# Second layer's first product by one level of Strassen's algorithm, with the output product one step behind

## The chip, the cores and the metric

The kernel runs on one core of a Trainium2 chip. A time is the device time in microseconds of one execution. The kernel before took 958.43 us (median of three runs, 956.42 to 958.74). TensorE is called PE, VectorE DVE, ScalarE ACT, GpSimd POOL and SyncE SP, as in the profile; PEld is PE's loading of weights.

## What is computed

A gated linear recurrence over 1536 tokens gives x (1536 x 320). A first layer multiplies it by w_in (320 x 2048), applies a piecewise quadratic function and multiplies by w_out. The second layer, with eight experts that all see all tokens, takes most of the time:

```python
logits = x @ w_gate                      # 1536 x 8
P = np.exp(logits - logits.max())
for _ in range(8):                       # Sinkhorn rounds
    P /= P.sum(1, keepdims=True) + 1e-09
    P /= P.sum(0, keepdims=True) + 1e-09
    P *= N / E
for e in range(E):
    h = np.maximum(x @ w1[e], 0.0)       # first product, 320 x 1024 weights
    out += P[:, e:e + 1] * (h @ w2[e])   # output product, 1024 x 320 weights
```

## The kernel before

Every float32 operand of a large product is held as two parts, hi (rounded to PE's fast 32-bit format) and lo (the rest), and a product is three products: hi x hi, lo x hi, hi x lo. ACT makes the hi parts, DVE or POOL subtract them from the values for the lo parts.

**First layer.** The tokens go in four groups g of 384. For each of 16 slices f of the hidden units PE runs `first_product` (L1221, eight matmuls of 384 columns, L1232) and, two slices behind, `second_product` (L1235, nine of 320 columns, L1242 and L1246). In between DVE clamps (L927), ACT squares (L534), DVE takes the larger (L952), ACT rounds to `ht_hi` (L415) and DVE or POOL make `ht_lo` (L940, L597). Between the slices of groups 0 to 2 stands attention work of the next group. After a group its outputs are copied to `xs`, transposed (`turn_mlp`, L1092) and split into `xt_hi` and `xt_lo`. In the last group PE also computes the router's logits of nine token tiles (`gate_logits`, L1268), and ACT and POOL already split the first expert's weights.

**Second layer.** Work goes by expert and by token group g of 512 (three). One `group` (L1361) on PE is: four times `hidden_pair` (L1334), each 30 matmuls of 512 columns that use 64 rows of the array, in pairs side by side (the 320 inputs are five pieces of 64; copies with swapped halves, `swap_hi` and `swap_lo`, put each piece also into the other half of the rows); then four times `output_tile` (L1348), each 24 matmuls of 320 columns for 128 tokens. ACT applies the relu from PSUM into `h_hi` (L568), DVE makes `h_lo` (L1033) and accumulates each output tile into `acc`, weighted by `prob` (L1050; L1045 for expert 0, whose sums are scaled later by L1041). POOL subtracts for the experts' weights only (`piece_lo_part`, L597). Weights arrive by 64 DMAs of 320 KB on SP's queue (`load_piece`, L316), each when a buffer of `raw` is free; the order on every engine is written out by hand, with semaphores between. The maximum of the logits and the eight Sinkhorn rounds (`sinkhorn_rows` L1000, `sinkhorn_columns` L1015 on DVE, `sum_columns` L1332 on PE) stand between the tiles of expert 0.

```python
for i, (w, x) in enumerate(parts):
    for j in range(2):
        half = slice(j * HALF, (j + 1) * HALF)
        ins = mm(ps_h2[pair % 2 * 2 + j][:, :], w[half, :], x[half, :], ...)
```

Of the kernel before, what the change touches and what calls it, by code (L numbers as in the profile page):

```python
# [22 lines left out]
GT = 3  # L23
# [18 lines left out]
EARLY = 6
SLOTS = 2
RESTS = 8
# [6 lines left out]
def column_round(g, t):  # L51

    r = (g - 1) * T2 + t
    return r if 0 <= r < SINKHORN else None
# [15 lines left out]
def build(nc, gates, select, qk, rows, up_down, rest, pieces, wgate, consts, factors, out):  # L70
# [18 lines left out]
    cst = sb("cst", [P, P + 1 + GH])  # L89
    ident = cst[:, 0:P]  # L90
    mask_up = cst[:, P:P + 1]
    onehot = cst[0:GH, P + 1:P + 1 + GH]
    all_ones = sb("all_ones", [P, P])
    xt_hi = sb("xt_hi", [P, 3, TOK], f32r)
    xt_lo = sb("xt_lo", [P, 3, TOK], f32r)
    before_hidden = mark[0]
# [15 lines left out]
    raw = sb("raw", [P, SLOTS, PU])  # L112
    after_raw = mark[0]
    mark[0] = raw_at
    st_hi = sb("st_hi", [P, RESTS, PS], f32r)
# [3 lines left out]
    wg2 = sb("wg2", [P, 3, 2, E], f32r)  # L119
    xs = sb("xs", [P, GT, 3 * P])  # L120
# [12 lines left out]
    e1_hi = sb("e1_hi", [P, NP2 * PU], f32r)  # L133
    e1_lo = sb("e1_lo", [P, NP2 * PU], f32r)
    h_hi = sb("h_hi", [P, FT2, GN2], f32r)
    h_lo = sb("h_lo", [P, FT2, GN2], f32r)
# [6 lines left out]
    assert mark[0] <= end_mlp  # L143
# [9 lines left out]
    e0_hi = sb("e0_hi", [P, NP2 * PU], f32r)  # L153
    e0_lo = sb("e0_lo", [P, NP2 * PU], f32r)
    swap_hi = sb("swap_hi", [P, 2, TOK], f32r)
    swap_lo = sb("swap_lo", [P, 2, TOK], f32r)
    assert mark[0] <= nc.sbuf_usable_end, (mark[0], nc.sbuf_usable_end)
    ex_hi, ex_lo = (e0_hi, e1_hi), (e0_lo, e1_lo)
# [35 lines left out]
    ps_gate = bank[0]  # L194
    ps_top = bank[1]
    ps_cols = bank[1][:, 2 * P:2 * P + E]
    ps_h2 = (bank[6], bank[7], bank[2], bank[3])
    ps_out2 = bank[4:6]
    ps_turn2 = (bank[6], bank[7], bank[2])
# [16 lines left out]
    piece_in = [mk(f"piece_in{i}") for i in range(SLOTS)]  # L216
    piece_hi = mk("piece_hi")
    piece_split = mk("piece_split")
    swap_in = [mk(f"swap_in{i}") for i in range(2)]
# [32 lines left out]
    wg_ready = mk("wg_ready")  # L252
# [31 lines left out]
    xm_hi = mk("xm_hi")  # L284
# [14 lines left out]
    h2 = mk("h2")  # L299
    hi2 = mk("hi2")  # L300
    lo2 = mk("lo2")
    out2 = mk("out2")
# [5 lines left out]
    waited = mk("waited")  # L308
# [3 lines left out]
    with block:  # L312

        @block.sync
        def _(sp):
            def load_piece(q, i):  # L316

                sp.wait_ge(piece_split, q + 1)
                sp.sem_inc(waited, 1)
                sp.dma_start(raw[:, i, :], pieces[ds(q, 1), :, :].rearrange("a p n -> p (a n)")).then_inc(piece_in[i], 16)  # L320
# [66 lines left out]
            def swap_halves(k, a, b):  # L387

                sp.wait_ge(xm_ready, after(b - 1))
                cols = slice(a * P, b * P)  # L390
                for x, y in ((xt_hi, swap_hi), (xt_lo, swap_lo)):
                    sp.dma_start(y[0:HALF, :, cols].bitcast(f32), x[HALF:P, 0:2, cols].bitcast(f32)).then_inc(swap_in[k], 16)
                    sp.dma_start(y[HALF:P, :, cols].bitcast(f32), x[0:HALF, 0:2, cols].bitcast(f32)).then_inc(swap_in[k], 16)

            sp.wait_ge(m_split, FT1)
            for q in range(NP2 - SLOTS):
                load_piece(q, q % SLOTS)
            swap_halves(0, 0, EARLY_X)
            for q in range(NP2 - SLOTS, NP2 + SLOTS):
                load_piece(q, q % SLOTS)  # L400
            swap_halves(1, EARLY_X, U)
            with sp.Fori((NP2 + SLOTS) // 2, E * NP2 // 2) as i:
                for j in range(2):
                    load_piece(i * 2 + j, j)
            for t in range(U):
                sp.wait_ge(acc_ready, after((E - 1) * U + t))
                row = t % B * S + t // B * P
                sp.dma_start(out[row:row + P, :], acc[:, t, :]).then_inc(stored, 16)
# [4 lines left out]
        def _(act):  # L413
# [3 lines left out]
            def piece_hi_part(q2, i, hi, c):  # L417

                act.wait_ge(piece_in[i], q2 * 16 + 16)
                copy(hi[:, c * PU:(c + 1) * PU], raw[:, i, :]).then_inc(piece_hi, 1)  # L420
# [91 lines left out]
            def copy_mlp(g):  # L512

                for t in range(GT - 1):
                    act.wait_ge(out1, g * GT + t + 1)
                    copy(xs[:, t, 0:DM], ps_out[t][:, 0:DM])
                    copy(xs[:, t, DM:3 * P], ps_out[t][:, 2 * P:DM]).then_inc(x2_act, 1)

            def turn_mlp_hi(g, banks=ps_out):
                for t in range(GT):  # L520
                    turn_hi(xm_turned, g * GT + t, banks[t], g * GN + t * P, xm_hi)

            def mlp(g, first, attention, piece):
                if not first:
                    copy_mlp(g - 1)
                for f in range(FT1 + 2):
# [9 lines left out]
                    if not first and f == 0:  # L536
                        turn_mlp_hi(g - 1)
# [13 lines left out]
            def expert0_piece_at(f):  # L551
                if f % 2 == 0 and f >= 2:
                    q = f // 2 - 1
                    if q == 0:
                        act.wait_ge(xa_ready, after(U - 1))
                    piece_hi_part(q // 2, q % 2, e0_hi, q)
# [4 lines left out]
            mlp(G - 1, False, False, expert0_piece_at)  # L561


            def group(ex, g, nxt, parts, first=False, exp_here=False):

                for f in range(FT2):
                    act.wait_ge(h2, (ex * G2 + g) * FT2 + f + 1)
                    nc.scalar.activation(h_hi[:, f, :], ps_h2[f % 4][:, :], ACT.Relu).then_inc(hi2, 1)  # L568
                    if exp_here and f == 0:
                        act.wait_ge(top_ready, 1)  # L570
                        nc.scalar.activation(prob[:, :, :], prob[:, :, :], ACT.Exp, bias=top[:, 2:3]).then_inc(probs, 1)
                if first:
                    turn_mlp_hi(G - 1, ps_turn2)
                if nxt is not None:
                    for c in parts[g]:
                        piece_hi_part((ex + 1) * (NP2 // 2) + c // 2, c % 2, ex_hi[nxt], c)

            copy_mlp(G - 1)
            for g in range(G2):
                group(0, g, 1, NEXT_FIRST, first=(g == 0), exp_here=(g == 1))  # L580
            for g in range(G2):
                group(1, g, 0, NEXT)
            with act.Fori(1, E // 2 - 1) as ep:
                for slot in range(2):
                    for g in range(G2):
                        group(ep * 2 + slot, g, 1 - slot, NEXT)
            for g in range(G2):
                group(E - 2, g, 1, NEXT)
            for g in range(G2):
                group(E - 1, g, None, NEXT)  # L590

        @block.gpsimd
        def _(pool):
# [3 lines left out]
            def piece_lo_part(q, i, hi, lo, c):  # L599

                pool.wait_ge(piece_hi, q + 1)
                cols = slice(c * PU, (c + 1) * PU)
                sub(lo[:, cols], raw[:, i, :], hi[:, cols].bitcast(f32)).then_inc(piece_split, 1)
# [61 lines left out]
            pool.sem_inc(piece_split, SLOTS)  # L665
# [70 lines left out]
            for ex in range(2):  # L736
                for c in range(NP2):
                    piece_lo_part(ex * NP2 + c, c % 2, ex_hi[ex], ex_lo[ex], c)
            with pool.Fori(1, E // 2) as ep:
                for slot in range(2):  # L740
                    for c in range(NP2):
                        piece_lo_part(ep * (2 * NP2) + slot * NP2 + c, c % 2, ex_hi[slot], ex_lo[slot], c)
# [4 lines left out]
        def _(dve):  # L747
# [5 lines left out]
            for s in (xa_ready, xm_ready, sink, acc_ready):  # L753
                dve.sem_inc(s, FREE)
# [161 lines left out]
            def turn_mlp_lo(g, banks=ps_out):  # L916
                for t in range(GT):
                    turn_lo(xm_hi, g * GT + t, banks[t], g * GN + t * P, xm_ready)

            def mlp(g, first, attention, lo, next_too):  # L920

                for f in range(FT1 + 2):
# [30 lines left out]
                    if f == 0 and not first:  # L953
                        turn_mlp_lo(g - 1)
# [8 lines left out]
                nc.vector.tensor_copy(xs[:, t, 0:DM], ps_out[t][:, 0:DM])  # L963
                nc.vector.tensor_copy(xs[:, t, DM:3 * P], ps_out[t][:, 2 * P:DM]).then_inc(x2_dve, 1)

            mlp(0, True, True, True, True)
# [99 lines left out]
            def no_gate(t):  # L1066
                pass
# [405 lines left out]
```

## Time and profile before

| | us |
|---|---|
| median of three runs | 958.43 |
| profiled execution | 956.86 |
| its span, first to last instruction | 955.1 |
| PE busy | 947.2 |
| DVE busy | 379.5 |
| ACT busy | 254.8 |
| POOL busy | 225.3 |

The profile is of one execution. Busy time is the sum of an engine's instructions; matmuls are pipelined, so the time from the start of one matmul to the start of the next (the spacing) is shorter than its duration. The chain that ended last is followed back from the last instruction, at each step to what released it.

### The profile page before, as it was taken

The page shows a single profiled execution, that of the slowest core. Times are in us where ns is not written, and L with a number is a line of the kernel's source. Part 1 is how long each engine was busy: PE and PEld are TensorE (multiplying, and loading weights), DVE is VectorE, ACT ScalarE, POOL GpSimd, SP SyncE. Part 2 cuts the span into 40 slices and gives each one's busy share as a digit, 9 for nine tenths or more (in the row PEclk, how much of TensorE's full clock was granted, in tenths as well). Part 3 has the DMA queues.
Part 4 walks back from the last instruction along what each step waited for, and adds up shares of the span by engine and source line. Part 5 has one row for each costly group of instructions (what it writes and reads, how often), then busy time and mean ns, then how long its engine had stood idle before and what let it go on. Part 6 is the DMA issues. An engine that isn't in the chain of part 4 may idle for free.

```text
span 955.1 us, 16999 instructions
## 1 busy us (share of the span) xinstructions
PE 947.2 (99%) x7157; PEld 866.3 (91%) x7157; DVE 379.5 (40%) x704; ACT 254.8 (27%) x498; POOL 225.3 (24%) x209
## 2 busy tenths in 40 slices
PE   9999999999999999999999999999999999999998
PEld 7799999999988989889999888999888999988998
DVE  6787665556432654333222222222222222222222
ACT  3544433335432212221212221122222112221111
POOL 5974555441210111110111110111110111110000
PEclk8999999999999999999999999999999999999999
DMA  8723224101611111000110001011001101100000
GB/s 297 228 68 110 76 67 123 43 2 42 154 32 45 42 43 42 27 16 29 42 42 29 28 15 42 29 42 42 29 12 31 42 28 43 41 2 1 29 28 28
DMA packets 29381, 50.38 MB, mean 53 GB/s; under 512 B 2416, under 2 KB 16864, under 8 KB 28928
## 3 DMA queue, kind: packets, MB, share of 16 engines
q1 hardware_dynamic: 28160, 43.59, 15.4%
q10 hardware_dynamic: 1152, 5.77, 1.6%
q8 instruction: 56, 0.92, 0.4%
q14 instruction: 13, 0.11, 0.0%
HBM read 44.15 MB, written 2.05 MB: 48 GB/s over the span
## 4 chain that ended last, share of the span: by engine, by line
PE 93%; DVE 3%; DMA 2%; ACT 1%; SPq 0%; issue 0%; DVEq 0%; ACTq 0%
PE bank L1344 35%; PE bank L1357 35%; PE bank L1232 9%; PE bank L1242 5%; PE bank L1246 3%; PE bank L1157 2%; DMA qk_s<-qk 1%; DMA factors<-dec 1%; PE bank L1130 1%; PE bank L1092 1%; PE bank L1151 1%; DVE ht_lo L940 1%; PE bank L1268 1%; PE bank L1147 0%; DVE h_lo L1033 0%
## 5 line engine op out<-in xcount | busy, mean ns | idle before, releaser
L1357 PE MATMUL bank<-e_hi,h_hi 128*128 128x320 f32 x768 | 241.0, 314 | 0.0
L1357 PE MATMUL bank<-e_lo,h_hi 128*128 128x320 f32 x768 | 237.4, 309 | 0.0
L1357 PE MATMUL bank<-e_hi,h_lo 128*128 128x320 f32 x768 | 237.3, 309 | 0.0
L568 ACT ACTIVATE h_hi<-bank 128x512 fp32r<-128x512 f32 x192 | 104.4, 595 | 469.8 <-PE bank L1344 469.8
L597 POOL TENSOR_TENSOR e_lo<-raw,e_hi 128x640 fp32r<-128x640 f32 x64 | 100.1, 1577 | 545.5 <-ACT e_hi L415 545.5
L1033 DVE SCALAR_TENSOR_TENSOR h_lo<-bank,h_hi 128x512 fp32r<-128x512 f32 x192 | 123.8, 686 | 244.8 <-ACT h_hi L568 244.8
L1357 PEld LDWEIGHTS bank<-e_hi,h_hi 128*128 128x128 f32 x768 | 144.2, 188 | 8.1 <-issue 8.0
L1357 PEld LDWEIGHTS bank<-e_lo,h_hi 128*128 128x128 f32 x768 | 144.3, 188 | 0.0
L1357 PEld LDWEIGHTS bank<-e_hi,h_lo 128*128 128x128 f32 x768 | 144.2, 188 | 0.0
L1050 DVE SCALAR_TENSOR_TENSOR acc<-bank,prob,acc 128x320 f32<-128x320 f32 x84 | 46.3, 551 | 216.5 <-PE bank L1357 216.5
L1344 PE MATMUL bank<-xt_hi,e_hi 64*128 64x512 f32 x576 | 118.0, 401 | 0.1
L1344 PE MATMUL bank<-xt_hi,e_lo 64*128 64x512 f32 x576 | 115.4, 391 | 0.0
L1344 PE MATMUL bank<-xt_lo,e_hi 64*128 64x512 f32 x576 | 114.9, 389 | 0.0
L1344 PE MATMUL bank<-swap_hi,e_lo 64*128 64x512 f32 x384 | 77.1, 392 | 0.0
L1344 PE MATMUL bank<-swap_hi,e_hi 64*128 64x512 f32 x384 | 76.9, 391 | 0.0
L1344 PE MATMUL bank<-swap_lo,e_hi 64*128 64x512 f32 x384 | 76.5, 389 | 0.0
L1344 PEld LDWEIGHTS bank<-xt_hi,e_hi 64*128 64x128 f32 x576 | 55.6, 184 | 15.3 <-issue 4.6
L1344 PEld LDWEIGHTS bank<-xt_hi,e_lo 64*128 64x128 f32 x576 | 55.8, 184 | 11.4
L1344 PEld LDWEIGHTS bank<-xt_lo,e_hi 64*128 64x128 f32 x576 | 55.8, 184 | 10.9
L927 DVE TENSOR_SCALAR vhalf<-bank 128x384 f32<-128x384 f32 x64 | 35.4, 553 | 63.8 <-PE bank L1232 62.3
L415 ACT ACTIVATE e_hi<-raw 128x640 fp32r<-128x640 f32 x64 | 45.0, 740 | 58.8 <-DMA raw<-pieces 58.8
L534 ACT ACTIVATE vhalf<-vhalf 128x384 f32<-128x384 f32 x64 | 33.6, 526 | 85.9 <-DVE vhalf L927 85.9
(134 smaller groups left out, 1139.1 us busy)
## 6 DMA issues: line engine op xcount, KB each, us to landing
raw<-pieces SPq DMA_DIRECT2D x64, 320.0 KB, 2.9
rw<-rows SPq DMA_DIRECT2D x12, 480.0 KB, 6.8
qk_s<-qk SPq DMA_DIRECT2D x12, 416.0 KB
fb<-factors SPq DMA_DIRECT2D x9, 512.0 KB, 5.9
m_raw<-up_down ACTq DMA_DIRECT2D x2, 1440.0 KB, 9.9
result<-acc SPq DMA_DIRECT2D x12, 160.0 KB, 1.8
decb<-factors SPq DMA_DIRECT2D x18, 80.0 KB
m_raw<-up_down ACTq DMA_DIRECT2D x1, 1152.0 KB, 11.2
```

Of the source, the lines that this page charges most:

```text
L415: return nc.scalar.activation(o, i, ACT.Copy)
L534: nc.scalar.activation(vhalf[:, f % 2, :], vhalf[:, f % 2, :], ACT.Square, bias=0.5, scale=0.5).then_inc(sq1, 1)
L568: nc.scalar.activation(h_hi[:, f, :], ps_h2[f % 4][:, :], ACT.Relu).then_inc(hi2, 1)
L597: return nc.gpsimd.tensor_tensor(o, a, b, ALU.subtract)
L927: nc.vector.tensor_scalar(vhalf[:, f % 2, :], ps_h[f % 2][:, 0:GN], -1.0, 1.0, ALU.max, ALU.min).then_inc(clamped, 1)
L1033: stt(h_lo[:, f, :], ps_h2[f % 4][:, :], 0.0, h_hi[:, f, :].bitcast(f32), ALU.max, ALU.subtract).then_inc(lo2, 1)
L1050: stt(acc[:, tile, :], ps_out2[t % 2][:, 0:DM], p, acc[:, tile, :], ALU.mult, ALU.add).then_inc(acc_ready, 1)
L1232: last = mm(dst[:, 0:GN], w, x, start=(i == 0), stop=(i == len(parts) - 1))
L1242: mm(ps_out[t][:, 0:DM], ht_hi[:, slot, t * P:(t + 1) * P], w[:, col:col + DM], start=(first and w is hi), stop=False)
L1246: ins = mm(ps_out[t][:, 0:DM], ht_lo[:, slot, t * P:(t + 1) * P], hi[:, col:col + DM], start=False, stop=last)
L1344: ins = mm(ps_h2[pair % 2 * 2 + j][:, :], w[half, :], x[half, :], start=(i == 0), stop=(i == len(parts) - 1))
L1357: ins = mm(ps_out2[t % 2][:, 0:DM], h[:, f, t * P:(t + 1) * P], w[:, col:col + DM], start=(f == 0 and i == 0), stop=(f == FT2 - 1 and i == 2))
```

## The change

Only the second layer and what leads to it are changed. For each pair of hidden slices (2 x 128 units) and each set of 768 tokens, the first product is a 2 x 2 by 2 x 2 block product: the 320 inputs as two halves of 160, the units as two of 128, the tokens as two of 384. Strassen's algorithm in Winograd's form takes seven block products instead of eight. There are 32 weight pairs and 2 token sets, 64 steps q.

- PE: `product(q, k)` is one block product, four matmuls of 384 columns: three with 128 rows and one with 96, in which the 32 leftover inputs of the three hi/lo combinations are stacked. `output_tile(q, t)` is six matmuls of 320 columns for 128 tokens. The tiles of step q-1 (and two of q-2) stand between the products of step q (`tile_after`).
- Weights: the four blocks of a pair come by one DMA of 512 KB, the output weights of the pair by one of 320 KB. POOL makes four weight sums (`pair_sums`), ACT the hi parts (`pair_hi`, `pair_rest_hi`, `pair_down_hi`), POOL the lo parts (`pair_lo`, `pair_down_lo`). There are three buffers.
- Tokens: x is kept as float32 (`xf`); seven operands for each token set are made once, by DVE (sums and lo parts), ACT (hi parts) and POOL (the leftover rows), during the last group of the first layer and the first three steps. The swapped copies and their DMAs go away.
- Results: the sums of block products are made in part by accumulating two products in a PSUM bank, in part by DVE (`drain`, five additions and one low part a step) and ACT (`first_sum`). The hidden lo parts of three of the four blocks move to POOL (`block_lo`), with ACT making the hi part and a relu copy for each (`block_hi`).
- Router: the logits are plain float32, all twelve tiles in steps 0 and 1; the maximum follows in step 2, the column sum of a Sinkhorn round every five products from (3, 4) on. `acc` is updated after each pair of slices instead of after each expert: 384 tile updates instead of 96.
- The transposes before the second layer have a fourth block each; ACT, DVE and POOL code is written out where it was in loops.

```diff
+A11, A12, A22, S3, S1, S2, S4 = range(OPS)
+B11, B21, T4, T3, T1, T2_, B22 = range(OPS)
+CHUNKS = (A11, S2, A12, S3, S1, A22, S4)
+ORDER = [(p, 0) for p in range(RING)] + [(p, 1) for p in range(RING)] + [(p, s) for p in range(RING, PN) for s in range(SETS)]
+SUMS_AT = [7 * 3 + 4 + 5 * r for r in range(SINKHORN)]
+
+def tile_after(q, k):
+
+    if k < 2:
+        return (q - 2, GT + 1 + k) if q >= 2 else None
+    if k < 6:
+        return (q - 1, k - 2) if q >= 1 else None
+    return None
...
+            def product(q, k):
+
+                p, s = ORDER[q]
+                o, w, b = CHUNKS[k], wu[p % RING], (0, 1, 0, 1, 2, 1, 2)[k]
...
+                if k == 3:
+                    pe.wait_ge(drained, DRAINS * q + DRAIN_S2)
+                if k == 4 and q >= 1:
+                    pe.wait_ge(drained, DRAINS * (q - 1) + DRAIN_C21)
+                if k == 5:
+                    pe.wait_ge(drained, DRAINS * q + DRAIN_S3)
+                if k == 6:
+                    pe.wait_ge(drained, DRAINS * q + DRAIN_C22)
...
+                x = xo[s][o]
+                parts = ((w[:, o, 0, :], x[:, 0, :]), (w[:, o, 0, :], x[:, 1, :]), (w[:, o, 1, :], x[:, 0, :]),
+                         (w[0:3 * HALF_K, o, 2, :], x[0:3 * HALF_K, 2, :]))
+                for i, (a, m) in enumerate(parts):
+                    last = mm(ring_bank(q, b), a, m, start=(i == 0 and k in (0, 1, 4)), stop=(i == len(parts) - 1),
+                              skip_group_check=True)
...
+            def output_tile(q, t):
...
+                if t == 0:
+                    pe.wait_ge(w_down, p + 1)
+                    pe.wait_ge(drained, DRAINS * q + DRAIN_C11)
+                    pe.wait_ge(low_ready, 3 * q + LOW_C21)
+                if t == GT:
+                    pe.wait_ge(low_ready, 3 * q + LOW_C12)
...
+            for q in range(QN):
+                for k in range(7):
+                    product(q, k)
+                    between(q, k)
+                    nxt = tile_after(q, k)
+                    if nxt is not None:
+                        output_tile(*nxt)
...
+            def pair_lo(p):
+
+                w = wu[p % RING]
+                pool.wait_ge(w_hi, p + 1)
+                for a, b in ((0, 4), (4, OPS)):
+                    sub(w[:, a:b, 1, :], raw_up[:, a:b, 0:P], w[:, a:b, 0, :].bitcast(f32))
+                for a, b in ((0, 4), (4, OPS)):
+                    last = sub(w[:, a:b, 2, :], raw_up[:, a:b, P:UP], w[:, a:b, 2, :].bitcast(f32))
+                last.then_inc(w_up, 1)
...
+            def block_hi(q, c, r, step, b):
+
+                act.wait_ge(drained, DRAINS * q + step)
+                nc.scalar.activation(h_hi[q % 2][b][:, :], c[:, :], ACT.Relu)
+                nc.scalar.activation(r[:, :], c[:, :], ACT.Relu).then_inc(relu_ready, 1)
...
+                if p == PAIRS:
+                    dve.wait_ge(sink, FREE + ROUND * SINKHORN)
+                    nc.vector.tensor_scalar(acc[:, unit, :], acc[:, unit, :], prob[:, unit, 0:1], None, ALU.mult).then_inc(scaled, 1)
+                dve.wait_ge(tiles, n + 1)
...
+            for q in range(QN):
+                for k in range(7):
+                    if k >= 1:
+                        drain(q, k)
+                    done = tile_after(q, k)
+                    if done is not None:
+                        accumulate(*done)
+                    between(q, k)
```

## Rows read from the trace of the kernel before

**Rows 1.** The page, parts 1 and 2: PE's busy time, and its granted clock in 40 slices.
```profile
PE 947.2 (99%) x7157; PEld 866.3 (91%) x7157; DVE 379.5 (40%) x704; ACT 254.8 (27%) x498; POOL 225.3 (24%) x209
...
PEclk8999999999999999999999999999999999999999
```

**Rows 2.** The chain that ended last: start us, length us, engine, output, line, count.
```profile
213.12 1.40 PE bank L1232 x8
...
263.57 14.12 PE bank L1344 x120
...
280.51 0.98 PE bank L1092 x9
...
316.40 3.62 PE bank L1357 x24
320.38 3.62 PE bank L1357 x24
...
370.04 14.27 PE bank L1357 x96
...
937.91 14.29 PE bank L1357 x96
```

**Rows 3.** Timeline of PE in the first layer: start us, length us, instructions.
```profile
187.27 0.60 PE L1242 MATMUL bank<-m_hi,ht_hi 128*128 128x320 f32 x3
...
188.59 0.51 PE L1232 MATMUL bank<-xt_hi,m_hi 128*128 128x384 f32 x2
...
189.98 0.60 PE L1242 MATMUL bank<-m_hi,ht_hi 128*128 128x320 f32 x3
```

**Rows 4.** Timeline of PE around one tile of router logits in expert 0.
```profile
289.57 0.31 PE L1357 MATMUL bank<-e_hi,h_lo 128*128 128x320 f32 x1
289.72 0.39 PE L1268 MATMUL bank<-wg,xt_hi 128*128 128x16 f32 x3
...
290.54 0.32 PE L1357 MATMUL bank<-e_lo,h_hi 128*128 128x320 f32 x1
```

**Rows 5.** Groups of instructions by line and shape: busy us, mean ns, idle before.
```profile
L597 POOL TENSOR_TENSOR e_lo<-raw,e_hi 128x640 fp32r<-128x640 f32 x64 | 100.1, 1577 | 545.5 <-ACT e_hi L415 545.5
L415 ACT ACTIVATE e_hi<-raw 128x640 fp32r<-128x640 f32 x64 | 45.0, 740 | 58.8 <-DMA raw<-pieces 58.8
L927 DVE TENSOR_SCALAR vhalf<-bank 128x384 f32<-128x384 f32 x64 | 35.4, 553 | 63.8 <-PE bank L1232 62.3 <-DMA factors<-dec 1.5
L415 ACT ACTIVATE ht_hi<-gact 128x384 fp32r<-128x384 f32 x64 | 33.6, 525 | 43.6 <-DVE gact L952 43.6
...
L597 POOL TENSOR_TENSOR ht_lo<-gact,ht_hi x32: 991/1018/1453, 99.2 to 211.0; 128x384 fp32r<-128x384 f32 x32
```

**Rows 6.** By line: duration min/median/max ns; and timelines of DVE and POOL.
```profile
L1041 DVE TENSOR_SCALAR acc<-acc,prob x12: 375/960/1710, 371.9 to 438.1; 128x320 f32<-128x320 f32 x12
...
L940 DVE TENSOR_TENSOR ht_lo<-gact,ht_hi x32: 541/554/5436, 39.2 to 261.9; 128x384 fp32r<-128x384 f32 x32
...
45.02 5.44 DVE L940 TENSOR_TENSOR ht_lo<-gact,ht_hi 128x384 fp32r<-128x384 f32 x1
...
48.61 1.43 POOL L597 TENSOR_TENSOR m_lo<-m_raw,m_hi 128x576 fp32r<-128x576 f32 x1
...
320.42 0.17 DVE L1017 TENSOR_SCALAR colinv<-bank 128x8 f32<-128x8 f32 x1
...
322.27 0.34 DVE L1012 TENSOR_REDUCE colpart<-prob 128x8 f32<-128x96 f32 x1
```

**Rows 7.** Timeline of PE's weight loads at changes between row forms.
```profile
183.09 0.97 PEld L1151 LDWEIGHTS bank<-st,qd 104*128 104x128 f32 x8
183.98 1.87 PEld L1157 LDWEIGHTS bank<-vi,at 128*128 128x128 f32 x16
...
511.94 0.19 PEld L1357 LDWEIGHTS bank<-e_hi,h_hi 128*128 128x128 f32 x1 [0.36 <-issue]
```

**Rows 8.** The page, part 6, DMA issues: KB each, median us to landing.
```profile
raw<-pieces SPq DMA_DIRECT2D x64, 320.0 KB, 2.9
```

More of the change, by code:

```diff
@@ L43 @@
 SLOTS = 2
+RING = 3
 RESTS = 8
@@ L385, in _ @@
                 load_unit(u)
[L387 to L404, printed above, removed]
+            sp.wait_ge(xa_ready, after(U - 1))
+            for p in range(PN):
+                load_pair(p)
             for t in range(U):
-                sp.wait_ge(acc_ready, after((E - 1) * U + t))
+                s = t // T2
+                q = QN - SETS + s
+                sp.wait_ge(acc_ready, q * T2 + t % T2 + 1)
                 row = t % B * S + t // B * P
@@ L560, in _ @@
                 mlp(g, False, True, lambda f: None)
[L561 to L590, printed above, removed]
+            mlp(G - 1, False, False, operands_at)
@@ new lines, in output_tile @@
+            def output_tile(q, t):
+                p, s = ORDER[q]
+                n, w = q * T2 + t, p % RING
+                if t == 0:
+                    pe.wait_ge(w_down, p + 1)
[3 more added lines that the diff above has]
+                    pe.wait_ge(low_ready, 3 * q + LOW_C12)
+                if n < RING:
+                    pe.wait_ge(xm_ready, (G - 1) * GT + n + 1)
+                else:
+                    pe.wait_ge(acc_ready, n - RING + 1)
+                half, cols = t // GT * 2, slice(t % GT * P, (t % GT + 1) * P)
+                hi, lo = h_hi[q % 2], h_lo[q % 2]
+                parts = [(h, w_, f) for f in range(2) for h, w_ in ((hi, wd_hi), (hi, wd_lo))]
+                parts += [(lo, wd_hi, f) for f in range(2)]
+                for i, (h, w_, f) in enumerate(parts):
+                    last = mm(ps_t[n % RING][:, 0:DM], h[half + f][:, cols], w_[w][:, f, :], start=(i == 0), stop=(i == len(parts) - 1))
+                last.then_inc(tiles, 1)
@@ new lines, in between @@
+            def between(q, k):
+                if q == 0:
+                    if k == 0:
+                        pe.wait_ge(wgate_in, 16)
+                    if k == 2:
+                        turn_mlp(G - 1)
+                    else:
+                        gate_logits(k if k < 2 else k - 1)
+                if q == 1 and k < 3:
+                    gate_logits(6 + k)
+                if (q, k) == (1, 6):
+                    for t in range(U - GT, U):
+                        gate_logits(t)
+                if (q, k) == (2, 4):
```

690 lines of the change are left out of this document (446 added, 244 removed).

## The prediction

> **What bounds the kernel now.** I read the busy shares first: TensorE (PE) is busy for 99% of the span and its granted clock is at the full 2.4 GHz level after the first slice [rows 1]. Busy time alone doesn't say that PE sets the end, so next comes the chain that ended last, in order of time [rows 2]. From 263.57 us on it is two blocks in turn: 120 matmuls of the first product (L1344) in 14.12 us, then 96 of the output product (L1357) in 14.27 us, 24 times, up to 937.91 + 14.29 = 952.20. So the second layer takes 688.6 us. 24 x 28.39 = 681.4 of it are those blocks; some 7 us are router work and small waits. The last group of the first layer runs from 213.12 to 263.57, 50.45 us. What counts is PE's spacing there, and whether the new feeding of PE keeps up.
>
> **Spacing of the new matmuls.** The change uses two forms that the first layer already runs side by side [rows 3]: eight matmuls of 384 columns take 189.98 - 188.59 = 1.39 us, 0.174 each, and nine of 320 columns take 188.59 - 187.27 = 1.32, 0.1467 each. Three waits lie in each such round and cost nothing visible. A block product is four matmuls of 384 columns (two full parts hi x hi and hi x lo, one lo x hi, and the 32 leftover rows of all three stacked in 96 rows), 0.695 us; an output tile is six of 320, 0.88 us. There are 64 steps (32 weight pairs x 2 token sets) of 7 products and 6 tiles: a step is 4.87 + 5.28 = 10.15 us.
>
> **PE's sum.** First product: 448 x 0.695 = 311.4 instead of 24 x 14.12 = 338.9. That is only 8%, not an eighth: the old form filled its rows completely (960 rows as 15 half-array parts, pairs side by side) in 60 x 512 columns a block, while the new one spends 4 x 128 rows on 480. Output product: 384 x 0.88 = 338.0; the old 24 x 14.27 = 342.5 also holds the changes between the half-array and the full form. One such change leaves a visible hole, the weight load at 511.94 starts 0.36 us after the one before it ended [rows 7].
>
> Router: a gate tile costs (290.54 - 289.57) minus two slots of 0.147, 0.68 us [rows 4]. Twelve now lie in the second layer (three before), and nine leave the last group of the first layer. They become plain float32: three calls instead of six, but float32 calls show two records each in this trace (the 16 of L1157 in rows 7 are 8 heads), so I keep 0.68; it could be 0.4 less or 0.7 more. Nine transposes take 0.98 us [rows 2], 0.11 each, twelve take 1.3. A column sum leaves a gap of 320.38 - 316.40 - 3.62 = 0.36 [rows 2], eight are 2.9; the maximum 0.5. Second layer: 311.4 + 338.0 + 12 x 0.68 + 1.3 + 2.9 + 0.5 = 662.3 against 688.6, that is -26.3. The first layer loses 9 x 0.68 = 6.1 and gains 3 x 3 x 0.11 = 1.0 for the fourth transpose of a tile (the last group's are in the 1.3). **PE alone: -31.4 us** (-26.3 - 6.1 + 1.0).
>
> **Can the others feed it.** Per step, by the rows' durations [rows 5]: VectorE does 6 drains (384 columns, one operand in PSUM, 0.55 us, 0.5 when the next follows at once) and 6 accumulations of the same size: 6.2 of 10.15 us. ScalarE: 0.203 + 0.84 us per 1000 columns fits 384 at 0.525 and 640 at 0.742, so 8 moves of 384 are 4.1 and a pair's weights (896, 896 and 640 columns) 0.95 + 0.95 + 0.74 = 2.6 every two steps: 5.4. GpSimd: 384 columns take 1.02 and 640 take 1.57, so 0.19 + 2.16 per 1000; a pair's four low parts 4.63, four weight sums of 256 columns 2.97, the down part 1.57, and six hidden low parts 6.1: 15.3 in two steps of 20.3, 75%. None is over PE in the steady part.
>
> The tightest chain is in every even step, in us from its start: third product ends 3.85, seen by ScalarE 4.0, first block 4.5, weights' high parts 5.5 and 6.5, GpSimd's low parts 11.2, then the hidden low parts of C22 12.2 and C21 13.2. The first output tile of this step is due at 10.15 + 3.85 = 14.0. Slack 0.8 us, so I cost it at nothing; if that cover is gone by x us more, it is 29 times (x - 0.8). The loads stand on SP's queue behind each pair's low parts: 512 KB for the up part, and 320 KB land in 2.9 us [rows 8]; by size up to 4.7, ready at 15.9, wanted by GpSimd at about 16.8. The odd steps have over 2 us. After the last product two older tiles come first (1.76 us), which hides the last chain; the end behind the last matmul stays at 2.9 us (955.1 - 952.2).
>
> **Where stalls come.** VectorE instructions that read and write SBUF alone, or take two SBUF operands, wait while GpSimd works. The scaling of acc takes 375 ns at best, 960 at the median, 1710 at worst; ht_lo has a median of 554 and once took 5.44 us while GpSimd worked without a pause, as in the row of 48.61 [rows 6]. GpSimd's busy share in the second layer goes from 15% (64 low parts, 100.1 us [rows 5], in 688.6) to 75%. Four places:
> - Sinkhorn, eight rounds within 36 products. One clean round is 322.27 + 0.34 - 320.42 = 2.2 us of VectorE [rows 6], with three instructions that meet GpSimd. I take 0.55 + 0.7 + 0.8 us of waiting at full GpSimd load, 1.8 (bounds 0 and 5.4). Per five products PE needs 5 x (10.15 / 7) + 0.36 = 7.6 us; VectorE 5 x 6.0 / 7 = 4.3, plus 2.2 + 1.8, is 8.3. In bursts the columns and rows stand in two neighbouring products, 4.2 + 1.8 against 3.15, with 1.9 us of lag allowed before PE waits for a drain. Both give about 0.7 to 1.0 a round: 8 us (0 to 34; at 5.4 it is 8 x 4.3).
> - Twelve scalings of acc at the fifth pair, in 12 tile slots of 1.57 us: drain 0.5, scaling 0.96, accumulation 0.55 are 2.0. 12 x 0.45 less the lag of 1.9: 4 us (0 to 12).
> - Last group of the first layer. VectorE does 1.65 us per slice of 2.71, and 13 of 18 slices get an operand sum (768 columns, at most 2 x 0.55, I take 0.95) or a low part (0.5); with 0.3 to 0.6 of waiting for each two-operand instruction it stands at about 2.7, just PE's pace, with some 2 us of lag allowed. 3 us (0 to 10). ScalarE's 1.05 us per slice ride in its idle time.
> - Steps 0 to 3: the operands of the second token set are made between drains, and rows wait for the exponential with its table load: 4 us (1 to 10). Longer copies before the three middle turns: 1 us.
> Stalls together 20 us, and **-31.4 + 20 = -11.4 us**.
>
> One rule of the Trainium skill speaks against this change: "SBUF — State Buffer", section "SBUF: two separate sides", calls the port pair that VectorE and GpSimd share an exclusive lock, held for a whole instruction, when the VectorE instruction has two SBUF inputs or runs in a two-port mode. The trace agrees in kind (375 to 1710 ns for one form), but the 5.44 us are more than one instruction's turn; by one turn at most (1.3 us for 512 columns), three times a round, the Sinkhorn stall would stay under 8 x (6.5 + 3.9 - 7.6) = 22 us instead of 34.
>
> **Rivals.**
> 1. Everything hides: VectorE catches up in its slack and stalls are 0 to 10 us. For it: before, only some 7 of 688.6 us were not blocks. Time -31 to -21: about 932. It wants waits under 1 us a round.
> 2. Slower: GpSimd's bursts starve VectorE. Place: Sinkhorn and the scalings; price by the 5.44 us row: 8 x 4.3 = 34, plus 12 for the scalings and 8 for the rest, 54 us, +23: 981. It decides from a mean wait of some 2.5 us a round: 8 x (2.5 - 1.1) + 12 + 8 are the 31.4. Against it: one such row stands beside many of one turn.
> 3. The even-step chain is late by 1 us more than its slack: +29 on the forecast, 976. Its durations are read from rows of contiguous tiles, the new ones are strided.
> 4. The 96-row matmul is treated as another form, as the half-array ones are. A change into the full form costs 14.27 - 96 x 0.1467 = 0.19 us; 896 changes are 170 us: about 1117. Against it: 8 loads with 104 rows (183.09, 0.97 us) are followed by full ones at the usual 0.11 [rows 7]. The page "TensorEngine Tiling (Array Packing)" of the Trainium skill, section "Tiling Modes", says that a change of mode drains TensorE and lists only 128, 64 and 32 rows as modes; by it 96 rows stay in the full one.
>
> **Numbers.** The span of 955.1 becomes 943.7; the profiled execution, 956.86 with 1.76 around its span, 945.5. It lies 1.57 under the median of the runs shown (958.43), so the time predicted for the median is 947.0. Chances: forecast (939 to 955.5) 0.44; rival 1 0.24; within 0.3% 0.10; rivals 2, 3 and milder mixtures of their stalls 0.18; rival 4 0.04. Faster by over 0.3% 0.68, within 0.10, slower 0.22; 0.3% is about what a measurement of this kernel tells from no change. The range takes in most of rival 1 and reaches up into rivals 2 and 3: 930 to 972.
>
> **What would show it.** Products spaced 0.695 and tiles 0.88 with 10.15 us a step after the sixteenth (a longer step that alternates: rival 3; a hole at every product: rival 4). PE waiting for drains on VectorE in steps 3 to 10, and there VectorE instructions of prob and acc at 0.7 to 2 us; at 5 us rival 2. The last group of the first layer at 45 to 50 us. The forecast is wrong if a wait in steady steps, which 64 steps multiply, is over 0.2 us.

## The result, and the profile after

The kernel before was timed again beside it.

| | before | after |
|---|---|---|
| median of the executions run side by side | 957.42 us | 933.57 us |
| profiled execution, its span | 956.86, 955.1 us | 935.04, 933.2 us |
| ratio of the times, 95% interval | | 0.975 [0.973, 0.978] |

The change makes the kernel 23.9 us faster; 11.4 were forecast. The time lies inside the range (930 to 972) and next to rival 1, "everything hides", at about 932.

The page of after, parts 1 and 2 (against [rows 1]), busy time by engine and TensorE's granted clock:

```profile
PE 922.8 (99%) x6081; PEld 908.4 (97%) x6081; DVE 629.3 (67%) x1194; ACT 436.8 (47%) x886; POOL 622.3 (67%) x639
...
PEclk8799999999999999999999999999999999999999
```

TensorE runs 1,076 instructions fewer and is still busy for 99%. The other three engines have gone from 40, 27 and 24% to 67, 47 and 67%, and TensorE doesn't show it. The clock stays at its full level after the first two slices.

The chain that ended last, in order of time: start us, length us, engine and line, count. It answers to [rows 2]; L1632 is the new block product, L1655 the output tile.

```profile
372.80 1.40 PE bank L1632 x8
374.20 0.88 PE bank L1655 x6
...
382.98 1.40 PE bank L1632 x8
...
923.23 7.05 PE bank L1655 x48
```

A step is 382.98 - 372.80 = 10.18 us; eight matmuls of 384 columns take 1.40, a tile of six 0.88. The span closes by three differences between the profiles (starts from TensorE's timelines):

| | before | after | difference | forecast |
|---|---|---|---|---|
| first product of the first layer's group 1 | 94.29 | 97.18 | +2.9 | 0 |
| from there to layer 2's first product | 169.21 | 165.31 | -3.9 | -5.1 + 4 = -1.1 |
| layer 2, to the last matmul's end | 688.70 | 667.79 | -20.9 | -26.3 + 16 = -10.3 |
| behind the last matmul | 2.9 | 2.9 | 0 | 0 |

Sum -21.9, as 955.1 became 933.2. TensorE's sum for layer 2 was 662.3; 667.79 stand there. The busy times by stretch say where the 5.5 us between them lie (start:end, length, then busy us of each engine with its instructions, granted clock, DMA share, GB/s):

```profile
262.49:299.00 36.51, 34.31 (x237) 33.59 (x236) 24.69 (x43) 20.04 (x44) 26.52 (x25) 1.00 0.16 48
299.00:366.00 67.00, 65.98 (x416) 65.18 (x416) 55.06 (x140) 31.60 (x61) 45.27 (x47) 1.00 0.11 31
366.00:920.00 554.00, 554.00 (x3485) 554.00 (x3484) 363.59 (x666) 263.10 (x512) 394.26 (x398) 1.00 0.14 41
```

2.2 us are lost in the first steps, 1.0 in the stretch of the Sinkhorn rounds, none in the 554 us behind. The other 2.3 us are longer issue, 1.9 of them the step, 64 x 0.03 us longer than summed. TensorE's waits in the whole of after, by line and releaser (total us, times, longest), name the idle time:

```profile
PE bank L1632 <- DVE s L1295: 2.1, 2, 1.6
PE bank L1526 <- DVE ht_lo L1174: 1.5, 3, 1.1
...
PE bank L1599 <- DVE top L1227: 0.6, 1, 0.6
PE bank L1603 <- DVE colpart L1247: 0.5, 1, 0.5
```

The 2.1 us of L1632 are 1.58 in step 1 and 0.50 at 349.99 us, between two Sinkhorn rounds; with L1599 (the maximum) and L1603 (the first column part) they are the 3.2 us of layer 2. Of L1526's 1.5 us, 1.3 lie in the head and 0.2 in the first layer behind it. The forecast had 16 us of stalls in layer 2 and 4 before it.

### The profile page after: what moved, and what is told of

Same layout as the page of the kernel before. It is cut to its first block, busy times and chain, and to the rows that moved or that the text cites. A ratio compares the mean times of both kernels' runs of the same rounds, so it can differ in the third digit from the quotient of the medians.

```text
span 933.2 us, 16313 instructions
## 1 busy us (share of the span) xinstructions
PE 922.8 (99%) x6081; PEld 908.4 (97%) x6081; DVE 629.3 (67%) x1194; ACT 436.8 (47%) x886; POOL 622.3 (67%) x639
## 3 DMA queue, kind: packets, MB, share of 16 engines
HBM read 50.45 MB, written 2.05 MB: 56 GB/s over the span
## 4 chain that ended last, share of the span: by engine, by line
PE 62%; DVE 0%; issue 0%; DVEq 0%
PE bank L1655 33%; PE bank L1632 30%; DVE acc L1279 0%; PE bank L1603 0%; DVEq L1271 0%
## 5 line engine op out<-in xcount | busy, mean ns | idle before, releaser
L1632 PE MATMUL bank<-xo,wu 128*128 128x384 f32 (+1 forms) x1792 | 377.8, 338 | 2.1 <-DVE s L1295 2.1
L1632 PEld LDWEIGHTS bank<-xo,wu 128*128 128x128 f32 (+1 forms) x1792 | 306.5, 188 | 2.8 <-DVE s L1295 2.6
L1279 DVE SCALAR_TENSOR_TENSOR acc<-bank,prob,acc 128x320 f32<-128x320 f32 x336 | 184.7, 550 | 143.2 <-PE bank L1655 141.7
L1655 PE MATMUL bank<-wd_hi,h_hi 128*128 128x320 f32 x768 | 232.6, 311 | 0.0
L1655 PE MATMUL bank<-wd_lo,h_hi 128*128 128x320 f32 x768 | 231.3, 309 | 0.0
L740 POOL TENSOR_TENSOR h_lo<-r,h_hi 128x384 fp32r<-128x384 f32 x192 | 193.5, 1025 | 54.5 <-ACT r L691 54.4
L740 POOL TENSOR_TENSOR wu<-raw_up,wu 128x512 fp32r<-128x512 f32 (+1 forms) x128 | 146.9, 1178 | 103.1 <-ACT wu L499 103.1
L1655 PE MATMUL bank<-wd_hi,h_lo 128*128 128x320 f32 x768 | 174.9, 309 | 0.0
L1655 PEld LDWEIGHTS bank<-wd_lo,h_hi 128*128 128x128 f32 x768 | 145.0, 189 | 0.0
L1655 PEld LDWEIGHTS bank<-wd_hi,h_hi 128*128 128x128 f32 x768 | 144.7, 188 | 0.1
L1655 PEld LDWEIGHTS bank<-wd_hi,h_lo 128*128 128x128 f32 x768 | 128.4, 188 | 0.0
## 6 DMA issues: line engine op xcount, KB each, us to landing
m_raw<-up_down ACTq DMA_DIRECT2D x2, 1440.0 KB, 10.3
```

The costliest lines, as they stand in the source:

```text
L740: return nc.gpsimd.tensor_tensor(o, a, b, ALU.subtract)
L1279: ins = stt(acc[:, unit, :], bank_, prob[:, unit, ex:ex + 1], acc[:, unit, :], ALU.mult, ALU.add)
L1632: last = mm(ring_bank(q, b), a, m, start=(i == 0 and k in (0, 1, 4)), stop=(i == len(parts) - 1), skip_group_check=True)
L1655: last = mm(ps_t[n % RING][:, 0:DM], h[half + f][:, cols], w_[w][:, f, :], start=(i == 0), stop=(i == len(parts) - 1))
```

## Experiments: what holds the time

In these texts "theory" is that TensorE's issue is the whole time and that the failed step is the stalls' size. Spans of layer 2 are taken as in the table above, first product to last matmul's end, since the head varies (next section).

**The head, after_again and before_again.** No edit.

> The changed kernel once more, for the parts that vary from one execution to the next. Both theories: 933.6 us, a steady step of 10.18 us. Open is the head: in the first profile of the changed kernel the first product of the first layer's second group starts 2.9 us later than before (97.2 for 94.3 us), with a lower granted clock from 20 to 40 us. If that belongs to the change it stands here again at 97 us or later; if it is chance it stands at 94 to 95.

> The kernel before once more. If the later start of the second group (97 for 94.3 us) belongs to the change, it starts at 94 to 95 us here; if the head only varies, it may start later here too.

Measured 933.83 and 958.58 us. Group 1 starts at 96.32 in after_again and 95.93 in before_again. TensorE's timeline there, of before, before_again and after:

```profile
94.29 0.52 PE L1232 MATMUL bank<-xt_hi,m_hi 128*128 128x384 f32 x2
```
```profile
95.93 0.51 PE L1232 MATMUL bank<-xt_hi,m_hi 128*128 128x384 f32 x2
```
```profile
97.18 0.52 PE L1512 MATMUL bank<-xt_hi,m_hi 128*128 128x384 f32 x2
```

The busy times from 20 to 40 us, of before, before_again and after (the 0.85 and 0.66 are the granted clock):

```profile
20.00:40.00 20.00, 18.78 (x125) 15.90 (x125) 11.98 (x23) 10.11 (x25) 17.08 (x17) 0.85 0.85 283
```
```profile
20.00:40.00 20.00, 19.79 (x111) 17.06 (x111) 10.46 (x21) 9.71 (x24) 14.95 (x16) 0.66 0.83 272
```
```profile
20.00:40.00 20.00, 19.80 (x114) 17.35 (x114) 10.54 (x25) 9.72 (x24) 15.64 (x19) 0.66 0.84 270
```

The unchanged kernel has the low clock and a later start too. Over the 14 profiles of after and its variants, which share this part, group 1 starts between 93.3 and 98.2 us, at 96.1 on average; the two of before, 95.1 on average, lie inside. So most of the head's +2.9 is the chance of one execution, and with two profiles of before a difference of about 1 us can't be told from it. What comes behind it repeats: 169.21 and 169.19 us of first layer before, 165.31 in both after; 688.70 and 688.79 us of layer 2 before, 667.79 and 667.80 after.

**eight.** One product more in each step:

```
+                if k == 0:
+                    for i, (a, m) in enumerate(parts):
+                        mm(ring_bank(q, b), a, m, start=(i == 0), stop=(i == len(parts) - 1), ...)
```

> Eight block products a step for seven: the first one is issued twice, the second time over the first, so the result stays and only TensorE's work grows by four matmuls of 384 columns a step. Theory (TensorE's issue is the whole time): 64 x 0.70 = 44.8 us more, 978.4, a step of 10.88, and 21 us slower than before. Rival (part of the steady step is feeding that the extra product would hide): less, 965 to 975.

Measured 978.42 us; ratio to before 1.022 [1.019, 1.024]. Layer 2 grows by 712.58 - 667.79 = 44.8 us, the whole of the issue time. The chain shows the extra product (L1633) between its neighbours:

```profile
509.11 0.70 PE bank L1635 x4
509.81 0.70 PE bank L1633 x4
510.51 0.70 PE bank L1635 x4
```

Nothing in the steady step hid any of it. With eight products in this form the kernel is 21.8 us slower than before (956.64 beside it). So the 44.8 us of the product that is saved are what makes up for the rows that four matmuls leave unfilled, and the rest of them is the gain.

**one_round.** `SINKHORN = 8` becomes 1; seven rounds are left out.

> Seven of the eight Sinkhorn rounds are left out. The forecast's sizes (1.8 us of waiting behind GpSimd a round, 8 us of stalls): the time falls by 7 x 0.36 us of column sums and by 7 us of stalls, to about 924. Theory now (waits of 0.8 us a round, as the changed kernel's trace shows, all but 1 us of them inside VectorE's slack): it falls only by the seven column sums and one short wait, about 3 us, to 930.5.

Measured 931.00; layer 2 665.20 for 667.79, so seven rounds cost 2.6 us in all. At the forecast's 0.36 us a column sum 2.5 of them are TensorE's own work. In after's trace one takes less: from product to product across a sum and a tile stand 337.32 - 335.53 = 1.79 us, and 338.92 - 337.32 = 1.60 across a tile alone, 0.2 us for the sum and 1.4 for seven. That leaves 1.2 us of stalls, of which one is visible, the 0.50 us at 349.99, which one_round doesn't have. The first round's wait of 0.5 us stays in both. The forecast's term was 8 us for eight rounds.

**no_scaling.** The line `tensor_scalar(acc[:, unit, :], ..., prob[:, unit, 0:1], None, ALU.mult)` and the wait on it go; the twelve scalings are left out.

> The twelve scalings of acc by the first expert's weight are left out, the accumulations that follow stay. The forecast's size (4 us of stalls): 929.6. Theory now (lag and slack hold them): no difference, 933.6 within 0.5 us.

Measured 933.75; layer 2 667.76, no difference. The busy times of 366 to 431 us, of after and of no_scaling:

```profile
366.00:431.00 65.00, 65.00 (x411) 65.00 (x410) 48.32 (x90) 30.41 (x59) 47.03 (x47) 1.00 0.15 44
```
```profile
366.00:431.00 65.00, 65.00 (x412) 65.00 (x411) 42.16 (x78) 30.41 (x60) 48.35 (x50) 1.00 0.15 46
```

VectorE (the third pair of numbers) loses 12 instructions and 6.2 us; TensorE is at 65.00 of 65.00 in both.

**pool_1 and pool_2: the even step's chain.** In `pair_lo`, ahead of its four low parts, for pairs from the fourth on:

```
+                for i in range(n if p >= 3 else 0):        # n = 1, 2
+                    sub(scratch[i][:, :, :], raw_up[:, 4:OPS, 0:P], w[:, 4:OPS, 0, :].bitcast(f32))
```

> GpSimd does one more low part of 384 columns (1.02 us), into scratch, ahead of the low parts of each of 29 weight pairs in even steps; all else stays. Forecast's slack of 0.8 us: 29 x 0.22 = 6.4 us more, 940. By the changed kernel's trace (the low part of C21 ends 1.15 us before its tile): no difference, 933.6 within 1 us.

> The same with two of them, 2.04 us. Slack 0.8: 29 x 1.24 = 36 us more, 969.6. Slack 1.15: 29 x 0.9 = 26 us more, 959.6, slower than before. If GpSimd's chain has more room than the trace shows: less than 15 us more.

Measured 938.69 and 964.66; layer 2 grows by 5.6 and 30.9 us, 0.19 and 1.07 for each of 29 pairs, so 0.83 and 0.97 us of slack. Part of this lies in single early waits (0.76 us at 320.86 in pool_1, behind a drain). In the steady steps every second one takes 10.31 us in pool_1 and 11.29 in pool_2 where it took 10.18, 0.13 and 1.11 more: slack 0.89 and 0.93. The forecast's 0.8 holds within 0.1; my 1.15, read off the changed kernel's trace afterwards, doesn't. pool_2 is slower than before (1.006 [1.004, 1.008]). TensorE's timeline there shows the due tile waiting in every second step:

```profile
497.52 0.39 PE L1658 MATMUL bank<-wd_hi,h_hi 128*128 128x320 f32 x1 [0.88 <-POOL h_lo L741]
...
503.21 1.56 PE L1635 MATMUL bank<-xo,wu 128*128 128x384 f32 x8
...
513.39 1.56 PE L1635 MATMUL bank<-xo,wu 128*128 128x384 f32 x8
...
518.96 0.39 PE L1658 MATMUL bank<-wd_hi,h_hi 128*128 128x320 f32 x1 [0.85 <-POOL h_lo L741]
...
524.65 1.56 PE L1635 MATMUL bank<-xo,wu 128*128 128x384 f32 x8
```

The starts of the eight-matmul blocks are 10.18 and 11.26 us apart, in turn. Beyond the slack of 0.9 us each further microsecond on this chain costs about 29 us: with 2 us more of GpSimd work a pair the change is a loss.

**no_lag.** Output tiles straight behind their own step's products:

```
             for q in range(QN):
                 for k in range(7):
                     product(q, k)
                     between(q, k)
-                    nxt = tile_after(q, k)
-                    if nxt is not None:
-                        output_tile(*nxt)
+                for t in range(T2):
+                    output_tile(q, t)
...
```

with VectorE's accumulations moved alike and ScalarE's high part of C12 at the end of its own step.

> Each step's six output tiles directly behind its own seven products, ScalarE's and VectorE's order changed to fit; all else stays. Theory: the chains behind C21 and C12 (drain 0.56, two relus 1.06, low part 1.0 us, one engine serving both) end 2.4 us after the last product in odd steps, and 6.3 us in even ones, where GpSimd has the next pair's low parts in front: 35 x 2.4 + 29 x 6.3 = 267 us more, 1200. Bounds: 64 x 2.4 = 154 more (1087) if the low parts don't get in the way. Rival (buffers and slack alone hide the chains, the lag isn't needed): within 10 us of 933.6.

Measured 1422.77 us, 223 more than expected. The timeline of two tiles and the busy times of a long stretch:

```profile
501.26 0.61 PE L1649 MATMUL bank<-wd_hi,h_hi 128*128 128x320 f32 x1 [5.63 <-POOL h_lo L739]
...
519.30 0.61 PE L1649 MATMUL bank<-wd_hi,h_hi 128*128 128x320 f32 x1 [4.49 <-POOL h_lo L739]
```
```profile
800.00:1400.00 600.00, 427.87 (x2139) 396.68 (x2140) 219.02 (x401) 162.14 (x318) 238.30 (x247) 0.82 0.08 23
```

TensorE waits 294.5 us in 63 places for GpSimd's low parts and 21 for VectorE's drains: 316, near the 267 expected, though the odd steps' 4.5 us are longer than my 2.4. Most of the other 171 of the 487 us by which layer 2 grew are slower matmuls: TensorE was granted 0.82 on average over those 600 us, a mixture of its levels of 2.4 and 1.2 GHz, where in after it has 1.00. From 429 to 1365 us it stands idle for mostly 4.5 and 5.6 us by turns, once a step, and goes on at the lower level. Behind the idle time that ends at 501.26, one tile's matmuls and then a later tile's:

```profile
501.93 0.47 PE L1649 MATMUL bank<-wd_hi,h_hi 128*128 128x320 f32 x1
502.20 0.47 PE L1649 MATMUL bank<-wd_lo,h_hi 128*128 128x320 f32 x1
...
507.45 0.31 PE L1649 MATMUL bank<-wd_lo,h_hi 128*128 128x320 f32 x1
507.60 0.31 PE L1649 MATMUL bank<-wd_hi,h_hi 128*128 128x320 f32 x1
```

The spacing is 0.27 us at a granted clock of 0.50 and 0.147 from 506.7 us on, at 1.00. Added up in windows of one microsecond, TensorE works 247 us of layer 2 at a granted clock under 0.55; at the full level that work would take 0.147 / 0.267 of the time, so 111 of the 171 us are there. The rest, windows of mixed clock and short gaps, was not divided. I had not priced any of it. The lag hides the chain, and with it keeps the clock.

## Experiments: how VectorE's waits behind GpSimd add up

**rounds_by3 and rounds_by2.** The 5 in `SUMS_AT = [7 * 3 + 4 + 5 * r ...]` becomes 3 or 2.

> The column sums of the Sinkhorn rounds stand three products apart instead of five. TensorE needs 3 x 10.18 / 7 + 0.36 = 4.7 us a round. Forecast's size (1.8 us of waiting): VectorE needs 3 x 0.86 + 2.2 + 1.8 = 6.6, eight rounds less 1.9 us of lag are 12.9 us more, 946.5. Theory now (0.8 us of waiting): VectorE 5.6, 8 x 0.85 - 1.9 = 4.9 us more, 938.5.

> The same, two products apart: TensorE 3.3 us a round. Forecast's size: VectorE 5.7, 8 x 2.4 - 1.9 = 17.6 us more, 951. Theory now: VectorE 4.7, 8 x 1.45 - 1.9 = 9.7 us more, 943.3.

Measured 935.99 and 947.93; layer 2 grows by 2.9 and 13.1 us. By three the small waits are nearer (4.9 expected, 12.9 by the forecast), by two the cost lies between the two. The groups of VectorE's three waiting forms (busy us, mean ns; clean they take 170, 260 and 260), in before, after and rounds_by2:

```profile
L1009 DVE TENSOR_SCALAR rowsum<-rowsum 128x12 f32<-128x12 f32 x8 | 5.7, 715 | 0.3
L1021 DVE SCALAR_TENSOR_TENSOR prob<-prob,colinv 128x96 f32<-128x96 f32 x8 | 4.0, 497 | 0.3
...
L1011 DVE TENSOR_TENSOR prob<-prob,rowinv 128x96 f32<-128x96 f32 x8 | 2.1, 258 | 0.3
```
```profile
L1246 DVE TENSOR_TENSOR prob<-prob,rowinv 128x96 f32<-128x96 f32 x8 | 4.1, 508 | 0.3
L1256 DVE SCALAR_TENSOR_TENSOR prob<-prob,colinv 128x96 f32<-128x96 f32 x8 | 4.0, 500 | 0.3
L1244 DVE TENSOR_SCALAR rowsum<-rowsum 128x12 f32<-128x12 f32 x8 | 3.9, 482 | 0.3
```
```profile
L1246 DVE TENSOR_TENSOR prob<-prob,rowinv 128x96 f32<-128x96 f32 x8 | 3.8, 473 | 0.3
L1256 DVE SCALAR_TENSOR_TENSOR prob<-prob,colinv 128x96 f32<-128x96 f32 x8 | 2.7, 341 | 0.3
...
L1244 DVE TENSOR_SCALAR rowsum<-rowsum 128x12 f32<-128x12 f32 x8 | 2.0, 249 | 0.3
```

A round waits 0.78 us in before, with GpSimd busy 14% of the time around (14.1 of 100 us), 0.80 in after, with it busy 68%, and 0.37 in rounds_by2. I had taken 2.05 at full load, 1.8 in the sum. GpSimd is busy for 42% of 299 to 332 us in rounds_by2 (13.75 of 33 us). So over these three the wait doesn't follow GpSimd's share. What does cost in rounds_by2 is not VectorE's work, 23.93 of 33 us there, but the round trip: TensorE stands for the column part (11.3 us in 8 waits, for 0.5 in after), and right behind it VectorE stands for TensorE's next tile:

```profile
311.30 0.26 DVE L1256 SCALAR_TENSOR_TENSOR prob<-prob,colinv 128x96 f32<-128x96 f32 x1
312.61 0.49 DVE L1275 TENSOR_TENSOR acc<-bank,acc 128x320 f32<-128x320 f32 x1 [1.06 <-PE bank L1655]
```

**probe, probe_swap and probe_2.** From step 12 on, short instructions of 12 elements in scratch behind VectorE's work of every product:

```
+                if q >= 12 and k % 2 == 0:
+                    nc.vector.tensor_scalar(scratch[:, at_ % 16, :], rowsum[:, :], 1e-9, None, ALU.add)
+                if q >= 12 and k % 2 == 1:
+                    tt(scratch[:, at_ % 16, :], rowsum[:, :], rowinv[:, :], ALU.mult)
```

probe_swap exchanges the two; probe_2 has two of the first form behind every product.

> From step 12 on one more short VectorE instruction behind every product, of 12 elements and SBUF to SBUF, by turns with one and with two SBUF inputs: how long do they wait while GpSimd is 71% busy? The forecast's sizes: 0.55 to 0.8 us of waiting each at full load, 0.4 to 0.55 us on average, and bursts of some turns: at 0.55 a step has 6.2 + 7 x 0.7 = 11.1 us of VectorE work in 10.18, and the time grows by 52 x 0.9 = 47 us. Theory now: 0.2 to 0.3 us on average, no more than one turn of GpSimd (1.3 us) as a rule, a step at 10.18 and the time at 933.6.

> The probe with its two forms exchanged: the two-input form behind the even products, the one-input form behind the odd ones. In the first probe the one-input form waited 0.62 us on average and the two-input form 0.20. If the place (what GpSimd does behind that product) sets the wait, the two means change sides: the two-input form now some 0.6, the one-input form 0.2. If the form sets it, they stay with their forms. Time 933.6 either way.

> Two short VectorE instructions of the one-input form behind every product from step 12 on. If every instruction waits its own turn, 0.43 us as in the probe before, whatever the engine's load, a step has 6.6 + 14 x 0.59 = 14.8 us of VectorE work and the time grows by 52 x 4.6 = 240 us, to 1175. If only the first of a pair waits: 6.6 + 7 x 0.59 + 7 x 0.16 = 11.9, 87 us more, 1020. If waits shrink when VectorE runs late (the wait ends with GpSimd's instruction, whenever VectorE came), a step stays at 10.18 and the time at 933.6.

Measured 934.08, 935.66 and 931.00 us; layer 2 is 667.80, 667.81 and 667.77, so the three times differ by their heads. The busy times of 386 to 906 us, of after, probe and probe_2, VectorE third:

```profile
386.00:906.00 520.00, 520.00 (x3271) 520.00 (x3270) 336.92 (x618) 250.07 (x487) 377.10 (x381) 1.00 0.14 42
```
```profile
386.00:906.00 520.00, 520.00 (x3271) 520.00 (x3270) 479.19 (x969) 243.88 (x487) 377.89 (x380) 1.00 0.14 41
```
```profile
386.00:906.00 520.00, 520.00 (x3271) 520.00 (x3270) 493.89 (x1325) 243.04 (x483) 377.93 (x379) 1.00 0.13 41
```

The first 351 instructions add 142.3 us to VectorE's row, 0.41 each. The next 356 add 14.7, 0.04 each: the waiting in all the probes falls from 151 us in probe (207.5 us for 352 instructions, less 0.16 each) to 115 in probe_2 (228.2 us for 708). So the forecast's size of one wait was right (the probes average 0.43 us over their clean 0.16), against my later 0.2 to 0.3; but waits don't add up. VectorE's row stood at 92 and 95% of the stretch, in probe a third of that waiting, and TensorE never stopped. The groups of probe and probe_swap:

```profile
L1343 DVE TENSOR_SCALAR scratch<-rowsum 128x12 f32<-128x12 f32 x201 | 155.0, 771 | 0.0
L1345 DVE TENSOR_TENSOR scratch<-rowsum,rowinv 128x12 f32<-128x12 f32 x151 | 52.5, 347 | 0.0
```
```profile
L1345 DVE TENSOR_TENSOR scratch<-rowsum,rowinv 128x12 f32<-128x12 f32 x201 | 154.9, 771 | 0.0
L1343 DVE TENSOR_SCALAR scratch<-rowsum 128x12 f32<-128x12 f32 x150 | 52.4, 349 | 0.0
```

The means stay with the place and leave the form. In the trace such a wait ends with the GpSimd instruction that runs when VectorE comes, so whoever comes later waits less. One of probe's longest, VectorE's row and GpSimd's (1.34 us up to 511.59, and 1.58 up to 511.57):

```profile
510.25 1.34 DVE L1343 TENSOR_SCALAR scratch<-rowsum 128x12 f32<-128x12 f32 x1
```
```profile
509.99 1.58 POOL L741 TENSOR_TENSOR wd_lo<-raw_down,wd_hi 128x640 fp32r<-128x640 f32 x1 [1.60 <-ACT wd_hi L490]
```

The longest of all the probes is 1.345 us, and GpSimd's instructions of 512 and 640 columns take 1.30 and 1.58. Here the trace agrees with the Trainium skill, page "SBUF — State Buffer", section "SBUF: two separate sides", for VectorE's side: of a GpSimd instruction and a VectorE instruction with two SBUF inputs or in a two-port mode, whichever starts first has the shared pair of ports for its whole instruction, and the other is blocked. The forecast cited it beside the sum and did its sum without it. The 5.44 us of [rows 6] don't fit: from 44.34 to 50.04 us GpSimd runs six instructions one behind the other, and VectorE's, which stands from 45.02 to 50.46, takes 0.54 clean, so it got no turn at the five changes between them. After has the same row, 5.43 us at 47.81. No run shows why.

**tuned.** The faster version, by order alone:

```
-SUMS_AT = [7 * 3 + 4 + 5 * r for r in range(SINKHORN)]
+SUMS_AT = [7 * 3 + 6 + 5 * r for r in range(SINKHORN)]
...
                 if (q, k) == (1, 2):
-                    operand_lo(10)
                     operand_sum(11)
+                if (q, k) == (1, 4):
+                    operand_lo(10)
...
-                if (q, k) == (2, 6):
+                if (q, k) == (3, 0):
                     spread_maximum()
```

VectorE's `negate_maximum` moves with the last, its first rows from (3, 2) to (3, 4).

> All work stays; three visible waits of TensorE are taken away by order alone: in step 1 the operand sum goes ahead of the drain of S3 without the low part that waited for ScalarE (1.6 us), the maximum is spread one product later (0.6), the rounds start two products later (0.5). Theory now, that visible waits on TensorE's row are all that is left besides its own issue: 2.7 us less, 930.9. Rival, that the next late thing takes their place: no difference, 933.6.

Measured 930.85, 3.0 us less than after_again beside it; ratio to before 0.972 [0.970, 0.974]. Layer 2 is 664.88, 2.9 less. The largest wait, in after, seen from TensorE and then from VectorE:

```profile
282.59 0.97 PE L1632 MATMUL bank<-xo,wu 128*128 128x384 f32 x4 [1.58 <-DVE s L1295]
```
```profile
279.55 0.83 DVE L1152 TENSOR_TENSOR xo<-tsum,xo 128x384 fp32r<-128x384 f32 x1 [1.18 <-ACT xo L516]
280.31 1.76 DVE L1140 TENSOR_TENSOR tsum<-xf,tsum 128x768 f32<-128x768 f32 x1
281.99 0.55 DVE L1295 TENSOR_TENSOR s<-bank,s 128x384 f32<-128x384 f32 x1
```

The low part stood 1.18 us for ScalarE, with the drain of S3, for which TensorE waits, queued behind it. In tuned it is gone, the maximum's wait too, and of the 0.50 us between the rounds 0.2 are left; the 0.5 us for the first column part stays.

## Why the prediction was right in kind and too small

**Right, by its own steps.** The spacing of the new matmuls: 0.70 and 0.88 us forecast as 0.695 and 0.88, a step of 10.18 for 10.15. TensorE's sum: 662.3 forecast, and tuned, with most waits gone, stands at 664.9, of which 1.9 are that 0.03. That 96 rows run like full ones (rival 4, 1117 us): no hole at any product. The even step's chain, costed at nothing with 0.8 us to spare: pool_1 and pool_2 measure about 0.9 in the steady steps, and rival 3's mechanism is real, 31 us for 2.04 us more. The other engines under their limits, and the tail.

**Wrong: the 20 us of stalls.** Their mechanism exists, their sizes don't:

- Sinkhorn, 8 us forecast: 1.0 us of idle TensorE in the stretch of the rounds; by one_round seven rounds cost 2.6 us with their column sums. Here the forecast fell. It took three waits of 0.55 + 0.7 + 0.8, scaled to full load, and put them on VectorE's queue like work. In after they are 0.80 together. With that, VectorE's 4.3 + 2.2 + 0.8 = 7.3 us stay below TensorE's 7.6, and no steady stall is due. The probes say why adding is wrong even where a wait is long: it shrinks as VectorE runs late.
- Twelve scalings, 4 us: none by no_scaling. The median of 0.96 us [rows 6] was again taken as work; after's own mean is 0.73.
- Steps 0 to 3, 4 us: 2.2 us of idle TensorE up to 299 us. It is a matter of order in VectorE's queue, and tuned took most of it away.
- The first layer, 3 + 1: 3.9 us were saved of the 5.1 of TensorE's sum, so 1.2 were lost; 0.2 of them are a visible wait, and no run divides the rest.

Together: 1.0 + 0 + 2.2 + 1.2 = 4.4 us of stalls for 20, and 2.3 us more of issue time, make all but 0.1 of the 13.4 us by which layer 2 and the first layer beat the forecast. The head gave 2.9 back in the profile that was compared. The medians differ by 23.9 us and the two spans by 21.9.

Rival 1 named this outcome and its condition, waits under 1 us a round, and [rows 6] with its 5.44 us kept me from it. That row is one of 32 and stands where GpSimd worked on weights without a pause; before's own rounds, 0.78 us each, were in the trace and had not been put together. Rival 2 decided from 2.5 us a round; no run came near it.

**Open.** What moves the start of group 1 between 93.3 and 98.2 us is not settled; the granted clock of 20 to 40 us alone isn't it, since probe_swap has 0.89 there and starts at 97.9. Nor was it tried how many more instructions VectorE can take before TensorE waits: probe_2 ends at 95%. Why one wait behind GpSimd took over 5 us is open too.

## What to carry to other kernels

Sum the issue time of the engine that is busy for 99%, and add stalls to it only where a queue's clean work, without its waits, comes near the budget. In the probes here a wait for another engine's running instruction ended with that instruction and shrank when the waiter was late: it used up slack and didn't add to the queue. Measure the slack of the tightest chain by lengthening it on purpose. Here 2 us more in every second step turn a gain of 2.5% into a loss, and without the one-step lag of the consumer the kernel takes half as long again.

## What the runs showed of the hardware

- Short VectorE instructions wait by place and not by form: 0.61 us behind even products and 0.19 behind odd ones (771 and 347 ns less 0.16), the same when the forms are exchanged.
- A second instruction right behind a waiting one costs VectorE's row 0.04 us on average; GpSimd's own durations don't change by it (1,016 and 1,024 ns for 384 columns).
- With idle time of mostly 4.5 and 5.6 us by turns, once a step, TensorE's granted clock was 0.82 in no_lag over 600 us, for 1.00 in after: 0.50 behind each such stop, with a tile's matmuls 0.27 us apart instead of 0.147. Work at 0.50 made at least 111 of no_lag's 487 us more.
- One VectorE subtraction of 384 columns took 5.44 us in before and 5.43 in after (clean 0.54) while GpSimd ran six instructions without a pause.
